# Scores of chunk 2 one fc1 step earlier, its bonus sums apart from them, and two GpSimd instructions exchanged

## The reference

```
state = 0
for t: cur = (u * k_t) outer v_t
       y_t = r_t @ (state + cur)
       state = w[:, None] * state + k_t outer v_t
```

## Time and profile before

| | |
|---|---|
| median of 3 runs | 417.05 us (416.99 to 417.21) |
| the profiled execution's own time | 416.61 us |
| its span | 414.9 us |
| PE busy | 406.4 us, 98% of the span |
| DVE / ACT / POOL busy | 242.5 / 188.3 / 231.6 us |
| granted TensorE clock, whole run | 0.999 of full speed |

### The profile page before, as it was taken

One profiled execution on the slowest core, in us unless ns is written; L12 is line 12 of the kernel. 1 busy time (PEld: TensorE's weight loads), 2 busy tenths in 40 slices (PEclk: granted clock), 3 DMA queues, 4 the chain that ended last, 5 costly groups with the idle time before them and its releaser, 6 DMA issues.

```text
span 414.9 us, 9131 instructions
## 1 busy us (share of the span) xinstructions
PE 406.4 (98%) x3537; PEld 391.1 (94%) x3537; DVE 242.5 (58%) x576; ACT 188.3 (45%) x409; POOL 231.6 (56%) x239
## 2 busy tenths in 40 slices
PE   8999999999999999999999999999999999999994
PEld 7799799999999999999999999999999999999994
DVE  7787855376576547654663487785635546364521
ACT  4786543233333333333343455552645455464420
POOL 3789865567856685668234336075083461825531
PEclk9999999999999999999999999999999999999999
DMA  7999996214030303020008001827382845729000
GB/s 261 402 396 358 352 374 239 74 45 146 13 118 2 138 21 118 2 87 21 2 18 345 2 1 40 323 79 239 133 315 91 341 154 209 293 86 362 4 33 28
DMA packets 18650, 64.97 MB, mean 157 GB/s; under 512 B 2204, under 2 KB 11718, under 8 KB 16433
## 3 DMA queue, kind: packets, MB, share of 16 engines
q1 hardware_dynamic: 16816, 59.68, 39.2%
q0 software_dynamic: 1792, 4.73, 3.0%
HBM read 51.98 MB, written 13.21 MB: 157 GB/s over the span
## 4 chain that ended last, share of the span: by engine, by line
PE 92%; DVE 3%; DMA 1%; issue 1%; POOL 1%; ACT 1%; SPq 0%; POOLq 0%; DVEq 0%
PE bank L1362 27%; PE bank L1364 26%; PE bank L1363 26%; PE bank L1380 3%; DMA rkt<-rkt 1%; PE bank L1409 1%; PE bank L1445 1%; PE bank L1449 1%; PE bank L1683 1%; PE bank L1438 1%; PE bank L1441 1%; PE bank L1536 1%; PE bank L1718 1%; PE bank L1719 1%; PE bank L1722 1%
## 5 line engine op out<-in xcount | busy, mean ns | idle before, releaser
L708 POOL TENSOR_TENSOR g_lo<-elu,g_hi 128x256 fp32r<-128x256 f32 x95 | 73.8, 778 | 86.8 <-ACT g_hi L875 86.2
L1362 PE MATMUL bank<-xt,wd_hi 128*128 128x256 f32 x285 | 80.5, 283 | 0.6 <-DVE elu L1190 0.6
L1364 PE MATMUL bank<-xt,wd_lo 128*128 128x256 f32 x285 | 80.4, 282 | 0.0
L1363 PE MATMUL bank<-xt,wd_hi 128*128 128x256 f32 x285 | 80.3, 282 | 0.0
L866 ACT ACTIVATE elu<-elu 128x256 f32<-128x256 f32 x96 | 40.1, 418 | 76.6 <-DVE elu L1182 76.0
L1362 PE MATMUL bank<-wd_hi,g_hi 128*128 128x392 f32 (+1 forms) x192 | 67.5, 351 | 0.0
L1364 PE MATMUL bank<-wd_hi,g_lo 128*128 128x392 f32 (+1 forms) x192 | 65.2, 340 | 0.0
L1363 PE MATMUL bank<-wd_lo,g_hi 128*128 128x392 f32 (+1 forms) x192 | 65.1, 339 | 0.0
L1190 DVE SCALAR_TENSOR_TENSOR elu<-elu,bank 128x256 f32<-128x256 f32 x96 | 40.3, 419 | 41.2 <-ACT elu L866 41.2
L875 ACT CAST g_hi<-elu 128x256 fp32r<-128x256 f32 x96 | 39.0, 406 | 43.8 <-DVE elu L1190 43.8
L1362 PEld LDWEIGHTS bank<-xt,wd_hi 128*128 128x128 f32 x285 | 53.9, 189 | 1.3 <-DVE elu L1190 1.1
(11 more groups left out here) (220 smaller groups left out, 944.8 us busy)
## 6 DMA issues: line engine op xcount, KB each, us to landing
we_raw<-wexp SPq DMA_DIRECT2D x8, 1536.0 KB, 6.8
wd_raw<-wexp SPq DMA_DIRECT2D x8, 1536.0 KB, 8.0
rkt<-rkt SPq DMA_DIRECT2D x12, 512.0 KB, 5.9
nat<-nat SPq DMA_DIRECT2D x9, 672.0 KB, 4.5
xrow<-slots SPq DMA_DIRECT2D x16, 193.0 KB, 7.0
wd_raw<-win SPq DMA_DIRECT2D x4, 768.0 KB, 9.4
wd_raw<-wout SPq DMA_DIRECT2D x4, 768.0 KB, 9.7
wo_tr<-wouttr SPq DMA_DIRECT2D x1, 3072.0 KB, 18.0
```

Of the source, the lines that this page charges most:

```text
L708: nc.gpsimd.tensor_tensor(g_lo[:, f % 4, :], elu[:, f % 2, :], g_hi[:, f % 4, :].bitcast(F32), ALU.subtract).then_inc(s_glo, 1)
L1362: mm(dst, w_hi, x_hi, start=start, stop=False)
L1363: mm(dst, w_hi, x_lo, start=False, stop=False)
L1364: return mm(dst, w_lo, x_hi, start=False, stop=stop)
```

## The change

`meeting(2)` becomes 1 where it was 2. The decay of chunk 2, which was counted from it, is set to 2 by name. The bonus sums of chunk 2 are no longer bound to its scores, they stand behind fc1 of step 2 in block 0. On GpSimd `queries(2)` comes ahead of `decay_state(1)`. In the plan of chunk 3, `before` is `meeting(2)`, so that its keys, queries, raw_bonus, with_u and sum stand on steps 2, 3, 4, 5 and 6 after the change; its diagonal, natural, decay, outer, back and state are set by name and stay.

```diff
--- before.py
+++ after.py
@@ -329,7 +329,7 @@
 
         def meeting(c):
 
-            return {2: 2, 3: 9, 4: FT + 1, 5: FT + 6, 6: 2 * FT - 3}.get(c, 2 * FT + 3 + 8 * (c - 7))
+            return {2: 1, 3: 9, 4: FT + 1, 5: FT + 6, 6: 2 * FT - 3}.get(c, 2 * FT + 3 + 8 * (c - 7))
 
         def plan(c):
 
@@ -337,7 +337,7 @@
             steps = {"scores": b, "decay": b + (2 if c > 4 else 0), "keys": before + 1, "queries": before + 2,
                      "mask0": b + (c > 4), "mask1": b + 1 + (c > 4)}
             if c == 2:
-                steps.update(diagonal=2, mask0=4, mask1=6, natural=7, outer=9, back=9, state=10, low=11)
+                steps.update(diagonal=2, decay=2, mask0=4, mask1=6, natural=7, outer=9, back=9, state=10, low=11)
                 del steps["keys"], steps["queries"]
             elif c < 5:
                 steps.update(rk=before + 3, with_u=before + 4, sum=before + 5, diagonal=before + 5, natural=before + 6)
@@ -668,8 +668,8 @@
             pool.wait_ge(s_sc, 4)
             pool.wait_ge(s_wlo, 2 * OCH)
             keys(2)
+            queries(2)
             decay_state(1)
-            queries(2)
             raw_pair(2)
 
             one = pool.alloc_register("one")
@@ -1584,7 +1584,7 @@
                     c = chunk_for("scores", n, f)
                     if c is not None:
                         scores(c)
-                    if c == 2:
+                    if n == 0 and f == 2:
                         bonus_sums(2)
                     c = chunk_for("back", n, f)
                     if c is not None:
```

## The result

The changed kernel takes 418.11 us (median of 10 runs, 417.63 to 419.12), the kernel before, timed beside it, 416.80 (10 runs). The ratio is 1.0035 (95% interval 1.0026 to 1.0044), that is 1.5 us more (1.1 to 1.8); the medians themselves are 1.3 apart. The forecast was +1.5 us, 418.5 with a range of 417.0 to 419.3.

What follows compares the result with a forecast made beforehand. TensorE sets the end; part 1's 0.3 us gain is swallowed by fc1 of step 9 starting 1.41 later, plus 0.11 for the long first distance: 1.5 us. Profiled 416.61 + 1.5 = 418.1, predicted 418.5 on the median's scale, range 417.0 to 419.3.

Steps and rivals of the forecast that it cites:

- Part 1: TensorE ahead of fc1 of step 2: scores of chunk 2 fill the wait, fc1 of step 3 comes 0.3 us earlier.
- with_u: GpSimd's product with u for chunk 3, now ahead of g_lo 6: ends at 34.5 us, before the change 36.04.
- From there to the ELU of step 7: VectorE needs 1.44 us after with_u for the sum, one subtraction and the ELU, which ends at 35.94.
- the gain of part 1 is swallowed: The 0.3 us gained upstream is lost at the wait ahead of fc1 of step 9, set by other engines' chain.
- Behind step 9 nothing is given back: After fc1 of step 9 TensorE goes on in the old rhythm; nothing later returns the 1.5 us.
- The loads of nat and u_nat: Chunk 3's loads land at 30.1 and 32.6 us, ahead of raw_bonus at about 31.1 and with_u at about 33.5.
- the picture of VectorE: Between the ELUs of steps 6 and 7: long idle time ahead of chunk 3's sum, which delays fc1 of step 9.
- The lower bound: GpSimd's pieces all at their shortest: with_u ends at 32.87, fc1 of step 9 at 34.36, 0.2 us of gain left.
- rival B: GpSimd, steps 3 to 6, gets fast enough: with_u ended by 32.8 gives -0.3, 416.75 us; chance 0.13.
- Rival C: The sum does not hold the ELU, only late g_lo count, at fc1 of steps 7 and 8: 417.35 us; chance 0.11.
- The charge of 0.35 us for each subtraction: GpSimd in the new stretch: five VectorE subtractions beside it add 0.35 us each, moving with_u from 32.87 to 34.62.
- 0.5 as the most: TensorE's hole ahead of fc1 of step 2: a perfect fill could give at most the hole itself, 0.5 us.

Runs made afterwards that it cites:

- the second experiment: The kernel before with only the five pieces of chunk 3 (keys, queries, raw_bonus, with_u, sum) a step earlier: ratio 1.0030 to the kernel before, +1.2 us.
- the memset experiment: The changed kernel with eight VectorE subtractions for the low parts of w_in and w_out replaced by memsets to zero: ratio 1.0006 to the kernel before, +0.2 us.
- the third experiment: The changed kernel with the sum of chunk 3 put back on step 7, behind the ELU of step 7: ratio 1.0019 to the kernel before, +0.8 us.
- the fuller fill: The changed kernel with chunk 3's five pieces on their old steps and the queries of chunk 2 on VectorE: ratio 1.0000 to the kernel before, 0.0 us.
- the sum alone on step 6: The changed kernel with keys, queries, raw_bonus and with_u of chunk 3 back on steps 3 to 6: ratio 1.0049 to the kernel before, +2.0 us.

## Why the prediction was right

The result lies on the forecast, and most of its steps hold. One does not, one thing was overlooked, and that the number came out so close is in part luck.

- Part 1. Predicted: scores at about 18.2, fc1 of step 3 earlier by 0.3. Measured, less the 0.40 of later start: 18.18 and 0.29.
- with_u. Predicted to end at 34.5 (34.3 and 34.6 by the two ways of reckoning). Measured 34.83 - 0.40 = 34.43.
- From there to the ELU of step 7. Predicted 1.44, measured 36.29 - 34.83 = 1.46, and fc1 of step 9 at 36.34 - 0.40 = 35.94 for a predicted 35.99.
- That the gain of part 1 is swallowed: shown by the second experiment, to within 0.07 us.
- Behind step 9 nothing is given back: right for 300 us; 0.2 us come back in the last experts.
- The loads of nat and u_nat don't hold anything: right, with 1.2 and 1.0 us of cover, and the memset experiment shows the second as the next bound.

Wrong was the picture of VectorE. I expected it to stand idle for long ahead of the sum, as in the 1.60 us of the earlier trace rows, and put the whole loss on the sum's place. It waited 0.25 us, and the new gap ahead of fc1 of step 9 is 0.75 us where the prediction wanted over a microsecond. Half of the loss (0.8 of 1.5) comes from the late g_lo, which delay the ELUs of steps 5 and 6, and from subtractions that wait for GpSimd. VectorE's own chain and GpSimd's thus ended 0.25 us apart, and reckoning by either would have given nearly the same ELU of step 7. That they met is luck. The lower bound (with_u at 32.87, then 0.2 us of gain) and rival B rest on with_u alone; with VectorE's work as it was, an early with_u would have given back 0.25 us and no more. Rival C described this part and put it at 0 to 0.6 net; it is 0.8 by the third experiment. Rival C and the forecast were two pieces of one chain, and the total came out right because the chain's end was reckoned from GpSimd's with_u, which does not ask how the delay is spread over the earlier steps. The charge of 0.35 us for each subtraction was also only half of the price. GpSimd paid 0.32 for each of the five (7.96 us where its pieces at their shortest make 6.35), and VectorE paid 0.39 itself (its five subtractions took 4.64 us where five of 0.54 make 2.70).

Overlooked was what bounds part 1 when it stands alone. The 0.3 us at fc1 of step 3 came, and 0.6 with the fuller fill, where the prediction had 0.5 as the most. But with chunk 3's plan as before only about 0.1 of either is left behind step 9, for GpSimd's natural of chunk 2 ends 0.14 us ahead of the outer that needs it. The prediction looked at GpSimd up to step 6; the natural is on step 7. The forecast was not touched by it: in the changed kernel GpSimd's pieces stand a step earlier, and the natural ends at 39.05, 1.26 us ahead of the outer at 40.31.

## What to carry to other kernels

A step number in a plan written by hand is often the base of others: before it is moved, list what is counted from it, here five pieces of the next chunk that cost 1.5 us where the move itself gained 0.3. A short piece that waits for another engine belongs behind the instruction that the bounding engine needs, not ahead of it. And where two engines slow each other, a microsecond taken off one is not a microsecond gained (0.4 of 0.8 here): look at whether the work of the other then falls beside it. Last, before filling a hole look at what the engine meets next: if another engine delivers something a little ahead of its need (0.14 us here), that little is all that filling a hole of 0.5 us can bring.

## What the runs showed of the hardware

- After a wait of TensorE of 2.08 us ahead of fc1 of step 9 (the sum alone on step 6) the granted clock fell from 1.00 to 0.50, its lower level of 1.2 GHz, for about 3 us of work (38 to 40 us whole, and parts of the microseconds before and after); the distance of matmuls of 256 columns went from 0.12 to 0.22 us. In the four other executions of that kernel the mean clock over the run shows no such fall. A distance of 0.93 us between starts in the changed kernel did nothing of the kind.
- The first matmul of 256 columns after a gap is followed by the next after 0.22 us and not 0.12 (36.34 to 36.56 in the changed kernel). Each gap costs this 0.1 us beside its length. A gap is not needed for it: behind the bonus sums, which end without one, the kernel before has 0.20 us (21.75 to 21.95).
- A VectorE copy of 128x8 numbers that starts 0.02 or 0.03 us after a GpSimd g_lo took 0.74 us in eight profiled executions and 0.16 in two.
